# VectorE transposes queries, scores and softmax in squares of 32x32; scores made transposed, on 128 partitions

## What is computed

```python
a = softmax(phi, axis=2)                       # over the 576 rows, per slot
k_m = np.einsum('bhsm,bhsd->bhmd', a, k)
v_m = np.einsum('bhsm,bhsd->bhmd', a, v)
scores = scale * np.matmul(q, k_m.transpose(0, 1, 3, 2))
attn = softmax(scores, axis=-1)                # over the 32 slots, eps 1e-9 in the sum
x = np.matmul(attn, v_m)                       # heads side by side: (4608, 512)
h = x @ w1_in;  x = np.where(h > 0, h, np.exp(np.minimum(h, 0)) - 1) @ w1_out
h = x @ w2_in;  x = (h * np.clip(h + 3, 0, 6) / 6) @ w2_out
```

## Time and profile before

| | us |
|---|---|
| median of 3 runs | 1591.58 (1590.13 to 1594.7) |
| the profiled execution's own time | 1593.15 |
| its span, first to last instruction | 1591.4 |
| TensorE busy | 1546.1 |
| VectorE busy | 645.8 |
| ScalarE busy | 648.6 |
| GpSimd busy | 133.4 |

### The profile page before, as it was taken

The page is one execution under the profiler, slowest core; times in us unless marked ns, Lnnn a source line. Parts: engine busy times, 40 slices in busy tenths (PEclk is TensorE's granted clock), DMA queues, the critical chain, the costliest instruction groups (busy, mean ns, idle before and its releaser), DMA issues.

```text
span 1591.4 us, 25313 instructions
## 1 busy us (share of the span) xinstructions
PE 1546.1 (97%) x10096; PEld 1363.4 (86%) x10096; DVE 645.8 (41%) x1163; ACT 648.6 (41%) x1363; POOL 133.4 (8%) x99
## 2 busy tenths in 40 slices
PE   4799999999999999999999999999999999999999
PEld 3698999989899898999988888878888888888887
DVE  3455555555555556554433222322222222322222
ACT  2565555555555555555742222222222222222222
POOL 0330000000000000000642010101001010101000
PEclk9799999999999999999999999999999999999999
DMA  9423222223222123204220101000010101010000
GB/s 244 127 65 68 53 62 51 54 55 68 53 66 63 29 64 68 53 16 148 75 89 0 54 1 54 0 27 28 0 53 2 54 0 54 0 55 1 27 1 27
DMA packets 178121, 79.91 MB, mean 50 GB/s; under 512 B 152400, under 2 KB 160592, under 8 KB 178000
## 3 DMA queue, kind: packets, MB, share of 16 engines
q1 hardware_dynamic: 168528, 76.07, 18.1%
q10 hardware_dynamic: 9472, 2.07, 0.9%
HBM read 59.24 MB, written 18.87 MB: 49 GB/s over the span
## 4 chain that ended last, share of the span: by engine, by line
PE 91%; ACT 3%; DVE 2%; issue 1%; ACTq 1%; SPq 1%; POOL 0%; DMA 0%; DVEq 0%
PE ps L263 29%; PE ps L265 28%; PE ps L264 28%; PE ps L319 2%; PE ps L290 2%; PE ps L335 1%; SPq L827 1%; PE ps L308 1%; DVE g L676 1%; ACT g L530 1%; ACT g L528 1%; DVE w_lo L668 1%; ACTq L591 0%; ACT w_hi L510 0%; PE ps L325 0%
## 5 line engine op out<-in xcount | busy, mean ns | idle before, releaser
L263 PE MATMUL ps<-g_hi,w_out_lo 128*128 128x288 f32 x1024 | 317.5, 310 | 1.3 <-POOL w_out_lo L755 0.7
L264 PE MATMUL ps<-g_lo,w_out_hi 128*128 128x288 f32 x1024 | 302.6, 295 | 0.0
L265 PE MATMUL ps<-g_hi,w_out_hi 128*128 128x288 f32 x1024 | 302.4, 295 | 0.0
L542 ACT ACTIVATE g<-ps,one_half 128x512 f32<-128x512 f32 x144 | 99.3, 690 | 470.0 <-PE ps L265 470.0
L689 DVE SCALAR_TENSOR_TENSOR g<-g,ps 128x512 f32<-128x512 f32 x144 | 99.1, 688 | 455.0 <-ACT g L542 455.0
L265 PE MATMUL ps<-x_hi,w_in_hi 128*128 128x512 f32 x576 | 224.1, 389 | 3.7 <-issue 3.7
L263 PE MATMUL ps<-x_hi,w_in_lo 128*128 128x512 f32 x576 | 224.1, 389 | 0.0
L264 PE MATMUL ps<-x_lo,w_in_hi 128*128 128x512 f32 x576 | 224.1, 389 | 0.0
L263 PE MATMUL ps<-w_out_hi,g_lo 128*128 128x512 f32 x576 | 224.1, 389 | 0.0
L264 PE MATMUL ps<-w_out_lo,g_hi 128*128 128x512 f32 x576 | 224.1, 389 | 0.0
L265 PE MATMUL ps<-w_out_hi,g_hi 128*128 128x512 f32 x576 | 224.1, 389 | 0.0
(11 more groups left out here) (108 smaller groups left out, 1905.6 us busy)
## 6 DMA issues: line engine op xcount, KB each, us to landing
layer_out<-y_sb SPq DMA_DIRECT2D x16, 576.0 KB, 3.4
x_raw<-layer_out SPq DMA_DIRECT2D x9, 1024.0 KB, 6.8
kv<-in_k SPq DMA_DIRECT2D x60, 144.0 KB, 3.4
kv<-in_v SPq DMA_DIRECT2D x60, 144.0 KB, 3.4
q<-in_q SPq DMA_DIRECT2D x60, 144.0 KB, 2.9
w_in_raw<-in_moe_w_in SPq DMA_DIRECT2D x8, 1024.0 KB, 11.5
w_out_raw<-in_moe_w_out SPq DMA_DIRECT2D x8, 1024.0 KB, 6.2
out<-out_sb SPq DMA_DIRECT2D x8, 1024.0 KB, 5.1
```

The lines of the kernel that those rows point to most:

```text
L263: nc.tensor.matmul(dst, a_lo, b_hi, start=first, stop=False)
L264: nc.tensor.matmul(dst, a_hi, b_lo, start=False, stop=False)
L265: return nc.tensor.matmul(dst, a_hi, b_hi, start=False, stop=last)
L542: nc.scalar.activation(g2[f % 2][:], hid(f, BLOCK), ACT.Relu, bias=one_half[:, 0:1], scale=1.0 / 6.0).then_inc(e_made, 1)
```

## The change

**Queries** come from memory in another layout: a partition holds, for one of four half-heads (two heads of a pair, two halves of 32 columns), row r of each of the 18 squares of 32 rows. VectorE transposes every square of 32x32 in one instruction over 128x576 and has the pair's queries transposed. TensorE's stages at steps 7 and 8 and both copies go. A load of queries has eight DMAs instead of four, with 32 partitions and 18 runs of 128 bytes each. VectorE waits for the load and for `kv_done` (the transposed queries lie where keys and values lay).

**Scores** are made transposed: four matmuls of 288 columns with the key memory of a pair of heads as weights (64 columns of the array), one pair on PSUM partitions 0 to 63 and the other on 64 to 127. VectorE transposes squares back from PSUM into `p`, 128 partitions by 18 squares by 32 slots; maximum, subtraction, exponential, sum and product run there, over 576 columns rather than 768.

**Softmax**: at step 14 VectorE transposes squares of `p` into `pT_raw` (which shares its place with `pT_lo`), ScalarE makes the high part from there, VectorE the low part. SyncE's load of phi waits for VectorE's transpose.

The first order shows TensorE ahead of unit 0, before and after: `q0` and `q1` are the two pairs' queries, `_b` is set B_, `kvm` holds the key memory, `rows` the softmax.

The diff, cut to its core:

```diff
+        pT_raw = [place(f"pT_raw{i}", [S], F32, at + i * PT_BYTES + S * 4) for i in range(4)]
...
-            t.q = [place(f"q{i}" + tag, [CH, 2, DH], F32, x) for i, x in enumerate(at_q)]
+            t.q = [place(f"q{i}" + tag, [TB, SQ], F32, x) for i, x in enumerate(at_q)]
+            t.p = place("p" + tag, [TB, M], F32, at_rows)
...
-        q_d = q.rearrange("b h (j p) d -> p (b h) j d", j=CH)
+        q_d = q.rearrange("b h (j r) (e c) -> e r (b h) j c", r=SQ, c=SQ)
...
-                elif stage in (S_Q0, S_Q1):
...
-                    for j in range(CH):
-                        mm = nc.tensor.transpose(chunk(t, j, ROWS), t.q[p][0:ROWS, j].rearrange("p h d -> p (h d)"),
-                                                 ident[0:ROWS, 0:ROWS])
-                    mm.then_inc(qT_done, 1)
                 elif stage == S_SCORES:
                     pe.wait_ge(kmT_copied, g + 1)
+                    pe.wait_ge(qT_made, nth(g, 1))
+                    for b in range(2):
                         for p in range(2):
                             lm = slice(p * 2 * M, (p + 1) * 2 * M)
+                            mm = nc.tensor.matmul(ps[lm, t.bank + b, 0:HALF], t.kmT[:, lm],
+                                                  t.qT[:, p, b * HALF:(b + 1) * HALF], start=True, stop=True)
                     mm.then_inc(scores_done, 1)
-                elif stage == S_PT:
...
                 elif f == 9:
+                    pe.wait_ge(kmT_copied, g + 1)
+                    pe.wait_ge(vT_made, g + 1)
                 elif f == 12:
+                    pe.wait_ge(p_sub_step, 3 * g + 1)
                 elif f == 15:
+                    pe.wait_ge(w1_lo_made, 2 * (2 * u + 4))
...
                 elif stage == S_PT:
+                    act.wait_ge(pT_made, g + 1)
+                    nc.scalar.copy(pT_hi[slot][:], pT_raw[slot][:]).then_inc(pT_hi_made, 1)
...
             for h in range(MAC):
+                for e in range(2):
+                    rows = slice((h % 2 * 2 + e) * SQ, (h % 2 * 2 + e + 1) * SQ)
+                    act.dma_start(B_.q[h // 2][rows], q_d[e, :, 2 * h + 1]).then_inc(B_.q_loaded[h // 2], 16)
...
                 elif stage in (S_Q0, S_Q1):
                     p = int(stage == S_Q1)
+                    dve.wait_ge(kv_done, g + 1)
+                    dve.wait_ge(t.q_loaded[p], 64 * nth_load(g))
+                    nc.vector.transpose(t.qT[:, p], t.q[p][:].rearrange("p j c -> p (j c)")).then_inc(qT_made, 1)
                 elif stage == S_SCORES:
                     dve.wait_ge(scores_done, g + 1)
+                    nc.vector.transpose(t.p_flat.rearrange("p (b c) -> p b c", b=2), t.ps_scores).then_inc(p_sub_step, 1)
...
                 elif stage == S_PT:
+                    dve.wait_ge(p_ready, g + 1)
+                    nc.vector.transpose(pT_raw[slot][:], t.p_flat).then_inc(pT_made, 1)
                     dve.wait_ge(pT_hi_made, g + 1)
...
             def loads_behind(g, follower, gi):
-                sp.wait_ge(qT_done, nth(g, 1))
+                sp.wait_ge(qT_made, nth(g, 1))
                 load_q(follower, gi, A)
                 sp.wait_ge(scores_done, g + 1)
                 load_kv(follower, gi, A)
-                sp.wait_ge(pT_done, g + 1)
+                sp.wait_ge(pT_made, g + 1)
                 load_phi(follower, gi, A)
```

More of the change, by code:

```diff
@@ L14 @@
 ROWS = 96
+SQ = 32
 MAC = 4
@@ L195, in build @@
             t.p_max, t.p_sum, t.p_sum_eps, t.p_inv = (
-                t.stats[0:ROWS, 3 + i * CH * MAC:3 + (i + 1) * CH * MAC] for i in range(4))
-            t.ps_cols = ps[:, t.bank:t.bank + 2, 0:CB * ROWS]
-            t.ps_rows = ps[0:ROWS, t.bank:t.bank + 2, 0:CB * P]
+                t.stats[:, 3 + i * TB:3 + (i + 1) * TB] for i in range(4))
+            t.ps_scores = ps[:, t.bank:t.bank + 2, 0:HALF]
             t.ps_kv = ps[:, t.bank, 0:2 * DH].rearrange("p (k c) -> p k c", k=2)
@@ L204, in build @@
             t.ps_vT = ps[:, t.bank + 1, P:2 * P]
[L205 removed]
             t.rows_flat = t.rows[0:ROWS].rearrange("p j c -> p (j c)")
[L207 to L214 removed]
+            t.p_flat = t.p[:].rearrange("p j m -> p (j m)")
         def kvm_block(t, h, gi):
@@ L427, in half @@
                             for e in (f - 1, f - 2):
-                                if e in items and stage in (S_MAX, S_KV, S_SCORES, S_PT):
+                                if e in items and stage in (S_MAX, S_KV, S_SCORES):
                                     behind = item_index(u, parity, items[e]) + 1
@@ L843, in load_q @@
                 for h in range(MAC):
-                    load(t.q[h // 2][0:ROWS, :, h % 2], q_d, head_of(g, gi, h), t.q_loaded[h // 2])
+                    for e in range(2):
+                        rows = slice((h % 2 * 2 + e) * SQ, (h % 2 * 2 + e + 1) * SQ)
+                        load(t.q[h // 2][rows], q_d[e], head_of(g, gi, h), t.q_loaded[h // 2])
             def load_in(i, layer, done):
```

75 lines of the change are left out of this document (17 added, 58 removed).

## The result

| | us |
|---|---|
| before, median of 4 runs | 1591.23 (1590.13 to 1594.7) |
| after, median of 4 runs | 1557.84 (1556.32 to 1558.73) |
| ratio, with its 95% interval | 0.978 (0.9768 to 0.9791) |
| span of the profiled execution, before and after | 1591.4, 1556.6 |

The change makes the kernel 2.2% faster. Forecast were 1566 us and a range of 1557 to 1578. The spans of the profiled executions differ by 34.8 us (the medians by 33.4) where the sum said 26.0. So 8.8 us came from somewhere that no term of the sum names.

The account below looks back on a forecast made before the run. TensorE, busy 97%, was taken as the bound. Queries 14.8, scores 12.2, softmax transposes with unit ends 0 and start -1.0 sum to 26.0 us, giving 1566 us on the median's footing, range 1557 to 1578.

Parts of the forecast that it names:

- Bound: Whole kernel: TensorE, busy for 97% of the span, bounds it; VectorE and ScalarE are busy for 41% each.
- Queries: Layer 1, steps 7 and 8: query transposes leave TensorE, hidden on VectorE at 0.75 us each; 14.8 us gained.
- rivals of dear squares: VectorE's square transposes: 1.15 us each gives 1573 us (chance 0.13); above 2.1 us the kernel is slower (0.05).
- The estimate from the Trainium skill's page: VectorE's square transpose: 311 ns for 128x128 bf16, taken as 2.4 ns a column, gives 1.40 us, total some 1578.
- Scores: Layer 1, 14 groups: four matmuls of 288 columns, halves side by side, cost 1.23 us; 12.2 us gained.
- halves in a row: Layer 1's scores: the four matmuls run one after another at 2.45 us, 17.1 us more, 1583 us; chance 0.09.
- Softmax transposes and even unit ends: Step 14 and even unit ends: 0.53 us gained and 0.8 lost, seven times, -1.9 us; softmax and ends together zero.
- The chain: Even unit ends: later transpose delays phi's load, VectorE's reduction and the accumulator copy; TensorE waits about 1.05 us where 0.27 was.
- Odd unit ends: Longer step 14 delays ScalarE's casts by about 0.4 us: 0.53 - 0.4, four times, +0.5 us; three others +1.6 us.
- Start: Before unit 0: eight query loads for four lengthen ScalarE's queue; first main matmul near 49.3 us; 1.0 us lost, ends 0 and +5.
- This later wait decides: Start: VectorE's wait for phi rows at 51.45 us, on SyncE's queue, moves by only 0.6 to 1.0 us and sets the loss.

Follow-up runs that it names:

- s_full: Changed kernel with each of the four score matmuls using all 128 array columns and writing all 128 partitions: 1570.77 us in one run.
- p_apart: Changed kernel with `p` of set A in a place of its own, so phi's load need not wait for VectorE's transpose: 1552.75 us, ratio 0.9745.
- a_pad66: Changed kernel with 66 more idle instructions (132 met waits) on TensorE ahead of its first matmul: 1568.6 us, ratio 0.9847.
- s_swap: Changed kernel with the score matmuls ordered pair by pair, two in a row writing the same half of the PSUM partitions: 1556.82 us, ratio 0.9769.
- start_act: p_apart with the second set's eight query loads issued on ScalarE behind its first two exponentials, not ahead of them: 1550.44 us, ratio 0.9731.
- b_pad80: Kernel before the change with 80 more idle instructions (160 waits) on TensorE at the start: 1590.66 us, ratio 0.9984.
- p_pad128: p_apart with 128 more idle instructions (256 met waits) on TensorE at the start: 1554.42 us, ratio 0.9746.
- unrolled: start_act with layer 1's loop written out for TensorE, ScalarE, VectorE and SyncE, GpSimd keeping its own: 1548.93 us, ratio 0.9722.

## Why the prediction missed, step by step

**Bound.** Right: TensorE at 97% before and after, and its timeline read from start to start gave every term that was looked for to within about 1.5 us.

**Queries.** Right in size (14.7 for 14.8) and in price (770 ns for 0.75 us). With them the rivals of dear squares fall. The estimate from the Trainium skill's page "VectorE: DVE Perf Modes", section "The three transpose paths" (1.40 us, from 311 ns for 128 columns), falls too: 770 ns were measured. That the page's figure holds a fixed part that does not grow with the columns would explain it; no run here has a transpose of another length.

**Scores.** Right in the mechanism: the two halves do run side by side, as the records' starts show, and s_full shows what it costs where they can't. From the first score matmul on an even unit's cost is the 1.23 us that was forecast; with the way to it from the last main matmul it is 1.32, so the term is 11.2 us and not 12.2. The rival "halves in a row" (2.45 us) falls. Its price was sound: at full width, where records do run one after another, s_full has 1.95 us in an even unit and 2.40 in an odd one.

**Softmax transposes and even unit ends.** The chain held, and p_apart shows it as cause. Forecast was 0.8 us more at each of seven even ends, 5.5 us; found were 0.10, 0.41, 0.71, 0.72, 0.65, 0.57 and 1.58 us over the 0.11 of before, 4.7 us. One link was off without harm: ScalarE's copy and not VectorE's is the late one. Two odd ends behind a loop's turn cost 0.75 and 0.98 us more, which was not seen coming.

**Odd unit ends.** Wrong: 0.4 us of later casts was charged to four ends. The plain odd ends cost 0.11 us after as before. TensorE does not wait for those casts, before or after: a delay of 0.4 us was charged without asking how long the cast had lain ready. That was 1.6 us too little gain.

**Start.** Too small: -2.0 us found for -1.0. (In the profiled executions of a_pad66 and s_swap, which start as the changed kernel does, it is -0.6 and -4.0, so this figure is only good to some 2 us.) "This later wait decides" was the step that failed. ScalarE's issues came to 12.11 us for 11.0 forecast and the first main matmul to 51.51 for 49.3, which is behind phi's landing. start_act shows that issues were the holder and phi's landing the next.

**No term for the loops' turns.** This is the step that put the time out of the range. The sum took everything outside the changed stages as fixed. It was in sight: TensorE's waits of before by releaser hold

```profile
PE ps L263 <- issue: 4.8, 2, 2.7
```

in layer 1 (us in total, times, longest) and 3.7 us in three in layer 2. The change takes 34 matmul records a group off TensorE (10096 to 9552 on the page), so its loops move, and those waits with them: 4.2 us in layer 2, shown by a_pad66, b_pad80 and p_pad128; and 2.4 us at layer 1's turns with 1.3 us of a lower clock behind one of them, for which the cause stays open. There b_pad80 stood longer than before did, by its place alone, but in the kernels built on the changed one the two waits lie between 1.1 and 1.8 us wherever the loop starts (1.30 and 1.40 in p_apart, 1.31 and 1.45 in p_pad128), and no rule found here foretells them. Terms and turns together make some 33 of the 34.8 us; about 1.5 us stays open. Had the rival "a standstill goes or comes" been written, with the 4.8 and 3.7 us that can be read from the trace of before, 8 us of either sign would have been in the range.

## What to carry to other kernels

Before a change that adds or removes many instructions is priced, look at every turn of every loop for idle time put down to "issue", and count it as free to come or go, also in loops that the change leaves alone. Where a load waits for the last reader of another tensor in the same place, try another place first: p_apart gained with one address nearly all that the new transposes had lost at unit ends. A gain at the start comes through only as far as the next load in the queue allows: here 5.3 of 7 us in the traces, and 2.3 in the medians.

## What the runs showed of the hardware

**Instructions are fetched in 16 KB pieces, and whether TensorE keeps a loop can hang on where it starts.** With 1576 instructions, layer 2's loop stayed from starts at 7, 57, 117, 218 and 245 of 256 and was fetched at each turn from 183, in two kernels, at 1.4 to 2.0 us of standstill each time. One constant offset of 38 to 72, which no run measures by itself, makes the former lie in seven pieces and the latter in eight. The Trainium skill, "Advanced Engine Details and Errata", section "ISA Cache", gives TensorE 128 KB in lines of 16 KB, 256 instructions each. The packets' size agrees (1.02 MB in 62). That would be eight lines; by this fit a loop over seven is kept and one over eight is not. It rests on a single place that was fetched, so it is an inference and not shown.

**VectorE can stand at its turn too.** In unrolled it stood 2.26 us at the turn of a loop of some 340 instructions. The same section gives the other engines 32 KB, two lines, which such a loop overruns from some places and not from others; no run here moved it to tell.

**Two fp32 matmul records that take half of the array's columns each run side by side.** For 288 columns both widths take 0.24 us from start to start; 64 wide there are two at a time, 128 wide one, with no effect of the order.

**A square transpose on VectorE** of 128x576 fp32 costs 770 ns, 1.34 ns a column with all that is fixed in it, and 9 ns more from PSUM: about as much as a subtraction of that size (758).

**DMA issues slow each other down.** An issue of keys took 0.65 us while little was queued and 1.5 us when both queues had many, one of queries 1.5 to 1.6 us; with a third queue in use from 1.6 us on, single issues of values took up to 3.1 us, and the first reduction of phi, which waits for its load, began 2.3 us later (8.73 for 6.42).
